# Fused local attention, gated mixing and a channel block on one core: spatial weights turned by VectorE, gate and projection later, the last v products first

## The reference

```
a = softmax(scale * q k^T + bias, masked to 8 global keys and a window of 96)   per head
x = a v                                      (B, S, 512), heads side by side

h = relu(x @ w_in)                           (B, S, 1024)
u, v = h[..., :512], h[..., 512:]
v_n = (v - mean(v)) / sqrt(var(v) + 1e-6)
v_s = einsum('ts,bsd->btd', w_spatial, v_n) + b_spatial      (mixes positions)
x = (u * v_s) @ w_out

h = x^T @ U @ V  (rank 32);  u = x + h^T
out = u + relu(u @ w_ch1) @ w_ch2            (hidden width 2048)
```

## Time and profile before

| | us |
|---|---|
| median of 3 runs (lowest, highest) | 562.88 (561.1, 563.14) |
| the profiled execution | 561.43 |
| its span, first to last instruction | 559.6 |
| TensorE busy | 525.5 (94%) |
| VectorE busy | 292.0 (52%) |
| ScalarE busy | 172.2 (31%) |
| GpSimd busy | 112.1 (20%) |

### The profile page before, as it was taken

The page is one execution under the profiler, slowest core; times in us unless marked ns, Lnnn a source line. Parts: engine busy times, 40 slices in busy tenths (PEclk is TensorE's granted clock), DMA queues, the critical chain, the costliest instruction groups (busy, mean ns, idle before and its releaser), DMA issues.

```text
span 559.6 us, 7557 instructions
## 1 busy us (share of the span) xinstructions
PE 525.5 (94%) x2676; PEld 409.6 (73%) x2676; DVE 292.0 (52%) x848; ACT 172.2 (31%) x426; POOL 112.1 (20%) x134
## 2 busy tenths in 40 slices
PE   1778999989999999999989999999999999999996
PEld 0455666567777788878768888888888888888885
DVE  4778888867775535689822265523146524011112
ACT  2665665555555533232311101021110102111010
POOL 3886000000000001499389500000000000000000
PEclk9999999999999999999989999999999999999999
DMA  8996453555514100055223100002000002000002
GB/s 176 220 222 131 101 103 90 119 113 131 127 48 123 29 29 1 1 170 166 79 75 114 37 1 0 1 0 76 0 1 1 1 0 77 0 1 0 1 0 81
DMA packets 43979, 37.04 MB, mean 66 GB/s; under 512 B 25600, under 2 KB 37888, under 8 KB 43936
## 3 DMA queue, kind: packets, MB, share of 16 engines
q1 hardware_dynamic: 37920, 20.13, 16.8%
q0 software_dynamic: 3216, 11.63, 6.8%
q10 hardware_dynamic: 2800, 4.72, 2.9%
HBM read 33.33 MB, written 3.15 MB: 65 GB/s over the span
## 4 chain that ended last, share of the span: by engine, by line
PE 80%; DVE 9%; DMA 3%; POOL 3%; issue 3%; ACT 1%; SPq 0%; DVEq 0%; POOLq 0%; ACTq 0%
PE ps L1185 66%; PE ps L1177 5%; PE ps L1225 4%; PE ps L1200 4%; DMA w_raw<-in_moe_w_in 3%; DVE uT_first L1003 2%; POOL win_lo L433 2%; PE ps L1316 1%; DMA qk_even<-in_q 1%; POOL win_hi L431 1%; DVE pr L875 1%; DVE uT_lo L1010 1%; DVE wspT_lo L962 1%; DVE gv_lo L943 1%; DVE sc L859 1%
## 5 line engine op out<-in xcount | busy, mean ns | idle before, releaser
L1123 DVE SCALAR_TENSOR_TENSOR hT_lo<-ps,hT_hi 128x512 fp32r<-128x512 f32 x48 | 33.2, 692 | 171.4 <-ACT hT_hi L731 171.4
L731 ACT ACTIVATE hT_hi<-ps 128x512 fp32r<-128x512 f32 x48 | 28.7, 598 | 228.3 <-PE ps L1185 228.3
L557 ACT ACTIVATE pr<-sc,small 128x256 f32<-128x256 f32 (+1 forms) x96 | 46.2, 483 | 52.5 <-DVE small L859 52.0
L1200 PE MATMUL ps<-k_turned,q_turned 64*128 64x256 f32 (+1 forms) x192 | 35.4, 448 | 16.5 <-DVE k_turned L811 10.0
L859 DVE CUSTOM_DVE_ANT_0 sc<-ps,bias 128x256 f32<-128x256 f32 (+1 forms) x96 | 34.9, 399 | 19.7 <-PE ps L1200 16.3
L1185 PE MATMUL ps<-win_hi,xT_hi 128*128 128x512 f32 x96 | 39.9, 416 | 0.0
L1003 DVE STREAM_TRANSPOSE ys<-tokens 32x128 f32<-32x128 f32 x128 | 38.7, 302 | 1.8
L1185 PE MATMUL ps<-uT_hi,w1a_hi 128*128 128x512 f32 x96 | 38.0, 396 | 1.0 <-DVE uT_lo L1010 1.0
L1185 PE MATMUL ps<-uT_hi,w1a_lo 128*128 128x512 f32 x96 | 38.1, 396 | 0.0
L1185 PE MATMUL ps<-uT_lo,w1a_hi 128*128 128x512 f32 x96 | 38.0, 396 | 0.0
L1185 PE MATMUL ps<-win_hi,xT_lo 128*128 128x512 f32 x96 | 37.7, 393 | 0.0
(11 more groups left out here) (146 smaller groups left out, 1078.0 us busy)
## 6 DMA issues: line engine op xcount, KB each, us to landing
w_raw<-in_moe_w_ch POOLq DMA_DIRECT2D x16, 512.0 KB, 4.0
wsp<-in_moe_w_spatial ACTq DMA_DIRECT2D x12, 384.0 KB, 3.5
vn<-in_v SPq DMA_DIRECT2D x12, 256.0 KB, 3.8
out<-ys SPq DMA_DIRECT2D x12, 256.0 KB, 3.3
qk_late<-in_q SPq DMA_DIRECT2D x24, 112.0 KB, 3.5
qk_late<-in_k SPq DMA_DIRECT2D x24, 112.0 KB, 3.9
vp<-in_v SPq DMA_DIRECT2D x10, 224.0 KB, 4.5
w_raw<-in_moe_w_in POOLq DMA_DIRECT2D x4, 512.0 KB, 7.1
```

What stands on the lines that cost most here:

```text
L557: act.activation(pr[:, k % 3, e, 0:w], sc[:, k % 2, e, 0:w], ACT.Exp, bias=nmax[:, k % 2, e:e + 1], scale=-1.0, accum_out=sums[:, k % 3, e ...
L731: act.activation(hT[0][:, n % 2, :], h1_ps(n), ACT.Relu).then_inc(s["hT_hi"], 1)
L1123: dve.scalar_tensor_tensor(hT[1][:, n % 2, :], h1_ps(n), 0.0, hT[0][:, n % 2, :], ALU.max, ALU.subtract).then_inc(s["hT_lo"], 1)
L1200: pe.matmul(scores_ps(e)[:, 0:w], q_turned[rows, tile % 2, p, :], keys[:, window_at(i):window_at(i) + w]).then_inc(s["scores"], 1)
```

## The change

- w_spatial is loaded in another layout: four transfers a tile (load_wsp), each of 32 partitions with 24 runs of 32 numbers (128 bytes), so that 32 x 32 block turns give its transpose. VectorE turns a half tile (128 x 384) with one instruction (turn_wsp) into wsp_turned, an SBUF tile that shares the place of wspT's low half. wsp_hi and wsp_lo read it there (SBUF minus SBUF, in place). TensorE's wsp_transpose is gone, and with it the PSUM banks that it used.
- In the second batch odd tiles have a home of their own for the raw and for the turned weights (wsp_late, wspT_late, wsp_turned_late), so loads run one tile further ahead.
- Freed banks: the transposed probabilities alternate between two until unit 31 (before: 24), x between two until tile 8 (PAIRED; before: 6).
- In the window stage TensorE makes gate_transpose after the second unit of a tile, and the projection after the third. VectorE's gT_lo stands behind its third unit, x2_lo behind its first, the turns of the next tile's weights on both sides of its second; ScalarE's lists follow.
- The v products of tiles 4 and 5 of batch 1 come first, then their u products (u_v_late).
- Tokens 0 and 1 are turned among the layer norms of batch 1 (eight turn_tokens calls), tokens 2 and 3 in products(1), two calls a tile instead of four; uT_hi and uT_lo come one tile earlier. In products(1) VectorE turns and splits the weights of tile t+1 ahead of gate t.
- finish(): hidden(0) goes ahead of the low rank product of tile 4.

```diff
-        wsp = sb("wsp", [P, S])
+        wsp = sb("wsp", [P, TURNS, NT, TURN])
...
-            return ps[:, 4 + (k % 2 if k < NT * NP else 0), :].rearrange("p (e c) -> p e c", e=2)
+            return ps[:, 4 + (k % 2 if k < ALONE else 0), :].rearrange("p (e c) -> p e c", e=2)
...
-            return ps[:, 6 + (tile % 2 if tile < NT else 0), :]
+            return ps[:, 6 + (tile % 2 if tile < PAIRED else 0), :]
...
+        def wsp_second(b, t):
+
+            return b == B - 1 and t % 2 == 1
...
-        wsp_d = w_sp.rearrange("(i p) s -> i p s", p=P)
+        wsp_d = w_sp.rearrange("(i r a) (k y c) -> i y r (a k) c", a=TURNS, r=TURN, y=TURNS, c=TURN)
...
-            def load_wsp(t):
-                act.dma_start(wsp[:, :], wsp_d[t, :, :]).then_inc(s["wsp_loaded"], 16)
+            def load_wsp(b, t):
+                for y in range(TURNS):
+                    act.dma_start(wsp_in(b, t)[y * TURN:(y + 1) * TURN, :, :, :].rearrange("p a k c -> p (a k) c"),
+                                  wsp_d[t, y, :, :, :]).then_inc(s[f"wsp_loaded{int(wsp_second(b, t))}"], 16)
...
+            def wsp_hi(b, t, h):
+                act.wait_ge(s["wsp_turned"], b * (2 * NT) + 2 * t + h + 1)
+                half = slice(h * HALF, (h + 1) * HALF)
+                act.activation(wspT_of(b, t)[0][:, half, :], wsp_turned_of(b, t)[:, half, :], ACT.Copy).then_inc(s["wspT_hi"], 1)
...
                 for t in range(NT):
                     a, after = ALONE + 3 * t, (t + 1) // NT
+                    exps(a + 2)
                     if t:
                         x2_hi(0, t - 1, False)
-                    exps(a + 2)
                     probs_out(a)
-                    gT_hi(0, t)
+                    if a + 2 > LAST:
+                        gT_hi(0, t)
                     exps(a + 3)
+                    wsp_hi(after, (t + 1) % NT, 0)
                     probs_out(a + 1)
-                    wsp_hi(after, (t + 1) % NT, 0, False)
+                    if a + 2 <= LAST:
+                        gT_hi(0, t)
                     exps(a + 4)
-                    wsp_hi(after, (t + 1) % NT, 1, False)
-                    load_wsp((t + 2) % NT)
+                    wsp_hi(after, (t + 1) % NT, 1)
+                    if t + 2 <= NT:
+                        load_wsp((t + 2) // NT, (t + 2) % NT)
...
+            def turn_wsp(b, t, h):
+                m = b * NT + t
+                half = slice(h * HALF, (h + 1) * HALF)
+                if h == 0:
+                    loads = sum(wsp_second(n // NT, n % NT) == wsp_second(b, t) for n in range(m + 1))
+                    dve.wait_ge(s[f"wsp_loaded{int(wsp_second(b, t))}"], 16 * TURNS * loads)
+                    dve.wait_ge(s["mixed"], m - 1 if b and t else m)
+                dve.transpose(wsp_turned_of(b, t)[:, half, :].rearrange("p k (r a) -> p a k r", a=TURNS),
+                              wsp_in(b, t)[:, :, half, :]).then_inc(s["wsp_turned"], 1)
...
+                dve.tensor_tensor(wspT_of(b, t)[1][:, half, :], wsp_turned_of(b, t)[:, half, :], wspT_of(b, t)[0][:, half, :],
+                                  ALU.subtract).then_inc(s["wspT_lo"], 1)
...
-                    gate(b, t, True)
-                    for h in range(2):
-                        if t + 1 < NT:
-                            wsp_lo(b, t + 1, h, True)
-                    for x in range(2):
-                        if b and t < TB:
-                            turn_tokens(t, x)
+                    if b == 0:
+                        gate(b, t, True)
+                    if t + 1 < NT:
+                        for h in range(2):
+                            turn_wsp(b, t + 1, h)
+                        for h in range(2):
+                            wsp_lo(b, t + 1, h)
+                    if b:
+                        gate(b, t, True)
+                        if t < TB:
+                            for g in (8 + 2 * t, 9 + 2 * t):
+                                turn_tokens(g // TURNS, g % TURNS)
                     if t:
                         x2_lo(b, t - 1, True)
                     gT_lo(b, t)
-                    for x in range(2, TURNS):
-                        if b and t < TB:
-                            turn_tokens(t, x)
-                    if b and t >= 2:
-                        uT_lo(0, t - 2)
+                    if b and 0 < t <= TB:
+                        uT_lo(0, t - 1)
...
+                    if k in (22, 24):
+                        turn_wsp(0, 0, (k - 22) // 2)
...
                 for t in range(NT):
                     a, after = ALONE + 3 * t, (t + 1) // NT
+                    unit(a, True)
                     if t:
                         x2_lo(0, t - 1, False)
-                    unit(a, True)
                     turn_next(a)
                     gate(0, t, False)
+                    turn_wsp(after, (t + 1) % NT, 0)
                     unit(a + 1, True)
-                    gT_lo(0, t)
+                    turn_wsp(after, (t + 1) % NT, 1)
                     turn_next(a + 1)
-                    wsp_lo(after, (t + 1) % NT, 0, False)
+                    if a + 2 > LAST:
+                        gT_lo(0, t)
+                    wsp_lo(after, (t + 1) % NT, 0)
                     if a + 2 <= LAST:
                         unit(a + 2, True)
+                        gT_lo(0, t)
                         turn_next(a + 2)
-                    wsp_lo(after, (t + 1) % NT, 1, False)
+                    wsp_lo(after, (t + 1) % NT, 1)
...
                     layer_norm(1, t)
+                    if t <= TB:
+                        for g in (2 * t - 2, 2 * t - 1):
+                            turn_tokens(g // TURNS, g % TURNS)
...
+            def u_v_late(b, t, wide):
+                for q in (0, 1):
+                    u_v_piece(b, t, q, wide)
+                for q in (2, 3):
+                    if t == NT - 1:
+                        u_v_piece(b, t - 1, q, wide)
+                for q in (2, 3):
+                    if t != NT - 2:
+                        u_v_piece(b, t, q, wide)
...
                 for t in range(NT):
-                    a, after = ALONE + 3 * t, (t + 1) // NT
+                    a = ALONE + 3 * t
                     mix_tokens(0, t, False)
                     unit(a)
-                    gate_transpose(0, t)
+                    if a + 2 > LAST:
+                        gate_transpose(0, t)
                     unit(a + 1)
+                    if a + 2 <= LAST:
+                        gate_transpose(0, t)
+                    if t == 1:
+                        wait(pe, "xT_lo", PAIRED)
                     if t:
                         low_rank(0, t - 1, False)
-                    wsp_transpose(after, (t + 1) % NT, 0, False)
-                    project(0, t, False)
-                    wsp_transpose(after, (t + 1) % NT, 1, False)
                     if a + 2 <= LAST:
                         unit(a + 2)
+                    project(0, t, False)
...
                 products(1)
-                wait(pe, "wspT_lo", 2 * B * NT)
+                hidden(0)
                 low_rank(1, NT - 2, True)
-                hidden(0)
                 project(1, NT - 1, True)
```

More of the change, by code:

```diff
@@ L63 @@
 CREDIT = dict(qk_turned=1, bias_ready=1, scores=1, biased=1, exps=4, normal=1, probsT=3,
-              pT_ready=2, av=1, xT_hi=1, xT_lo=2, d_xT_lo=3, v_relu=2, u_relu=2, wsp_transposed=1, wspT_lo=2, gate=2,
+              pT_ready=2, av=1, xT_hi=1, xT_lo=2, d_xT_lo=3, v_relu=2, u_relu=2, gate=2,
               gT_lo=1, x2_split=2, low_rank=2, mix_split=1, h_ps=1, u_ready=2, h1_ps=1,
@@ L175, in program @@
         wspT = hi_lo("wspT", [P, NT, P])
+        wspT_end = place[0]
+        place[0] = wspT_at + NT * P * 4
+        wsp_turned = sb("wsp_turned", [P, NT, P])
+        assert place[0] == wspT_end
         vf_at = place[0]
@@ L298, in program @@
             xT_hi xT_lo uv v_done u_relu v_relu stats_ready meanvar_ready var_ready rstd_ready normed
-            gv_hi gv_split wsp_transposed wspT_hi wspT_lo mixed gate gate_transposed gT_hi gT_lo
+            gv_hi gv_split wsp_turned wspT_hi wspT_lo mixed gate gate_transposed gT_hi gT_lo
             x2_sum x2_hi x2_split low_rank mix_hi mix_split h_ps u_ready
@@ L754, in _ @@
         def _(dve):
-            give(dve, "qk_turned", "bias_ready", "biased", "normal", "xT_lo", "d_xT_lo", "wspT_lo", "gate", "gT_lo",
+            give(dve, "qk_turned", "bias_ready", "biased", "normal", "xT_lo", "d_xT_lo", "gate", "gT_lo",
                  "x2_split", "mix_split", "u_ready", "hT_lo", "y_ready")
@@ L1051, in every @@
                     for h in range(2):
-                        wsp_lo(b, 0, h, True)
+                        turn_wsp(b, 0, h)
+                    for h in range(2):
+                        wsp_lo(b, 0, h)
                     for t in range(NT):
                         layer_norm(b, t)
+                        if b and 0 < t <= TB:
+                            for g in (2 * t - 2, 2 * t - 1):
```

(35 more changed lines are left out.)

73 lines of the change are left out of this document (44 added, 29 removed).

## The result

The changed kernel takes **570.9 us** (570.3 to 572.0, four runs) beside 562.7 us of the kernel before: ratio 1.0153, 95% interval 1.0128 to 1.0178. It is slower by 1.5%. The profiled execution took 570.92 us, span 569.1.

What follows compares the result with a forecast made beforehand. From 118.5 us on the kernel was taken as a chain of TensorE instructions, where only TensorE time and pauses count. The terms, -1.5 + 7.1 + 0 + 0.9 = +6.5 us, gave 568.5 us, range 560 to 576.

Steps and rivals of the forecast that it cites:

- term 2: Before the first mix at 118.5: xT_lo wait and transposes go, VectorE gets two turns; -1.5 us (-2.7 to 0).
- term 5: Second batch's products: 6.9 us of transposes and waits removed, 7.8 us added; +0.9 us (-6.9 to +7).
- term 3: First batch's products: waits for VectorE and a late load add 10.75 us, transposes remove 3.6; +7.1 us (0 to +16).
- Term 1: TensorE's weight transposes removed: 0.6 us a tile, 3.6 us in the first batch's products, 2.4 us in the second's.
- Term 4: Second batch's u and v products: VectorE gets 10 us of token turns and is full; TensorE's time changes by 0.
- (a): Second batch's products: last gv_lo late by VectorE's full queue in the u and v stage, 1.5 us (0 to 3.5).
- (b): Second batch's products: gate 0 stands behind two turns and two wspT_lo of tile 1; TensorE waits 2.7 us.
- (c): Second batch's products: wspT_lo, both operands in SBUF, blocked by GpSimd's splits, 1.3 us a tile; gated waits of 3.6 us.
- Clock: Second batch's products: half clock behind the x_lo and uT_lo waits moves behind two new waits, 0 (-1.5 to +2).
- (A): Second batch freed, not slower, if VectorE's list stays under TensorE's 8.0 us a tile: -2.8 us, 559.3; chance 0.2.
- (B): Loads of short runs late in every tile, not tile 0 alone: 7 us more, 576 us; chance 0.13.
- (C): Nearly cancels: turns take 0.55 us, little blocking; first batch's products +4, second's -1.5, in all +1: 563.5 us; chance 0.12.

Runs made afterwards that it cites:

- e1: Changed kernel with the first batch's gate transposed after a tile's first unit and projected before its third, gT_lo ahead of the second turn: 562.8 us, ratio 1.0013.
- e4: Changed kernel with each tile's raw weights loaded as before, one transfer of 3 KB rows (output not the reference's): 570.3 us, ratio 1.0153.
- e7: Changed kernel with the first batch's gate transposed and gT_lo taken early, but the projection still behind the third unit: 569.8 us, ratio 1.0141.
- e6: As e5, with two of the eight token turns moved from the second batch's layer norms into its products: 556.4 us, ratio 0.9895.
- e3: Changed kernel with the turned weights of the second batch's tiles 1 to 5 in PSUM instead of SBUF: 565.7 us, ratio 1.0063.
- e5: Changed kernel with the edits of e1 and e3 together: 558.3 us, ratio 0.9913.
- e8: Kernel before with only the second batch's last two v products put ahead of their u products: 560.0 us, ratio 0.9957.
- e10: Kernel before with only the first batch changed, in the order of e1: 557.8 us, ratio 0.9926.

## Why the prediction was right, step by step

The forecast was 568.5 us and slower; 570.9 is 2.4 above it and inside the range. The mechanism held in both places; several sizes were off. By the traces the change adds 9.5 us where my terms summed to 6.5 (8.2 by the medians): term 2 came out 0.5 too hopeful and term 5 3.0 too low, term 3 was 0.7 too high, and inside the terms too much and too little partly cancelled, which is luck.

**Term 1, the transposes' price, 0.6 us a tile: too low.** Tile 2 of e1, without a wait in either kernel, takes 13.28 us where it took 14.00 (e1's mixes start at 145.64 and 158.92): 0.72. In the second batch, the stage's 67.0 us are the 63.1 of before, less 4.4 us of waits that it had, plus 10.6 of new ones and 1.6 of half clock, which leaves 3.9 for the transposes where I had 2.4. That is a remainder, but five tiles at 0.72 make 3.6. Together they were worth about 2 us more than my 6.0.

**Term 2, -1.5 us: -1.0 in the table, sign and mechanism held.** From TensorE's pause at 91 us, which both traces have, to the first mix it is 27.5 us before and 26.15 in the changed kernel (118.52 - 91.04 and 117.51 - 91.36), -1.3. The wait of 2.0 us for xT_lo is gone, as forecast. A wait of 0.5 us for the scores, right ahead of the mix, is new and took back part of the relief; that VectorE's two turns cause it is not shown, they stand at 91.6 and 98.4.
The four rows, before and then changed:
```profile
91.04 0.63 PE L1177 MATMUL ps<-ident,pr 128*128 128x128 f32 x4 [0.48 <-issue]
...
118.52 0.50 PE L1185 MATMUL ps<-gv_hi,wspT_hi 128*128 128x512 f32 x1
```
```profile
91.36 0.63 PE L1247 MATMUL ps<-ident,pr 128*128 128x128 f32 x4 [0.48 <-issue]
...
117.51 0.50 PE L1255 MATMUL ps<-gv_hi,wspT_hi 128*128 128x512 f32 x1
```

**Term 3, +7.1 us: +6.4 measured, and tile by tile.** Beside the kernel before the tiles took +5.1, +0.1, +0.1, +0.2, +1.6 and -0.8 us; the forecast was +4.7 (3.2 + 0.9 + 1.2 - 0.6), +0.35 twice, +0.65, +1.7 and -0.6. The projection of tile 1 was put at M + 7.25 and came at M + 7.19. Tile 4 is right to 0.1. Tile 0's size is right in good part by luck. The wait for the scores was 0.85 smaller than forecast, and 1.6 us of half clock behind the waits of 2.35 and 0.73 were not in the sum. The raw weights, to which I gave 1.2 us, were not late at all: VectorE's turn follows gated at once, and each of the four transfers landed a median 3.5 us after its issue, where I had 6.7 for the tile. The new load does cost tile 0 1.2 us, as e4 shows, but through ScalarE's queue, whose issuing I had put at 0. And e7 shows that I named the lesser of two causes: I worked out when gT_lo comes, but not that the projection, moved behind the third unit, no longer covers that unit's operands.

**Term 4, 0: held.** The stage took 34.6 us in both. VectorE's time went from 17.9 to 23.3 us there.

**Term 5, +0.9 us: +3.9 measured.** This is where the forecast fell short.
(a) The last gv_lo was to cost 1.5 us (0 to 3.5). It cost 1.26 + 3.46 = 4.7, outside my bounds. From VectorE's first addition to its last gv_lo it is now 31.2 us where it was 27.3. VectorE is busy for 26.7 of them, close to the 27.1 that I had summed; the other 4.5 us are the short waits of each layer norm, which I named and did not put into the size. Both last steps of the chain are slow, vnf 1.24 us (0.55 in the other tiles) and gv_lo 2.05 (0.68), beside GpSimd's first splits. But they were as slow in the kernel before, 1.24 and 2.09, so they are no part of the difference. e6 took half of this wait away by moving two token turns, which shows the queue's part. The stretch in the changed kernel and its vnf, then the vnf of the kernel before:
```profile
217.03:248.23 31.20, 26.54 (x116) 21.32 (x114) 26.71 (x65) 7.98 (x14) 8.28 (x8) 0.96 0.00 1
...
244.25 1.24 DVE L993 TENSOR_SCALAR vnf<-vf,small 128x512 f32<-128x512 f32 x1 [0.44 <-POOL small L485]
```
```profile
234.84 1.24 DVE L950 TENSOR_SCALAR vnf<-vf,small 128x512 f32<-128x512 f32 x1 [0.44 <-POOL small L455]
```
(b) Gate 0: 2.7 us forecast, 3.6 measured. The turns cost what I said (1.5), the two wspT_lo 3.2 instead of 1.0, as my own part (c) should have told me.
(c) The block by GpSimd: 1.3 us a tile forecast, 9.3 us in five tiles measured, 1.9 each. The mechanism is the one I named, and e3 shows it by moving one operand. Four tiles are blocked, by 1.9 to 3.0 us, and the fifth hardly, and the mean of wspT_late_lo is 1216 ns, well over 0.55, as was said to show it. The waits for gated of tiles 1 to 3 came to 2.3 us and not 3.6: I had put TensorE's list at 8.0 us, and half clock made it longer, 3.2 us of extra time in this stage, which may be the reason; no run tells. The block is the rule of the Trainium skill, page SBUF — State Buffer, section Who interferes with whom, which the forecast cited: the traces agree, with 3.17 us for a pair beside a split and 1.02 for the same pair with an operand in PSUM. The forecast's way without that rule would have missed by 3.6 us more.
Clock: I had taken the loss as moved, 0 (-1.5 to +2). Fourteen products and the first transposes of gated ran at half clock, 3.2 us, against some nine products, 1.6 us, before: +1.6.
So the sum of term 5 was short by 2.8 us of waits and 1.6 of clock, and the transposes gave back 1.5 more than it had: 0.9 + 2.8 + 1.6 - 1.5 = 3.8.

**The rivals.** (A), the second batch freed, needed less than 0.5 us blocked a tile; it was 1.9. With that block gone and the first batch in e1's order the changed kernel is faster than the one before: e5 by 4.9 us, e6 by 6.8. (B), loads of short runs, is refuted by e4: 0.6 us in all, within the noise. The page DMA: Bandwidth & Descriptors of the Trainium skill, Specifications, stood on its side; the packets do cost the DMA engines twice the time, but the queues had room. (C) had the sign of the sum and no more: a turn takes 0.75 us and not 0.55, and its term 5 was to be -1.5.

**What was said to show it.** Mixes every 14.12 and 14.14 us in tiles 1 and 2 (14.2 forecast), with 0.65 us for gT_lo (0.95); in tile 3, which I had put beside them, 14.55. Scores in tile 0: 2.35 (3). No wait of VectorE for raw weights, against one in tile 0: wrong. gv_lo and gated head the waits of the second batch; the first hidden product waits for nothing: both right.

## What to carry to other kernels

When work moves from the bound engine to one with room, ask what now stands between each pair of its results and their use: here, with the same turns, the first batch's products took 6.4 us more than before or 1.3 less, by whether gT_lo and the 2.85 us projection stood ahead of the third unit's work or behind it. Look at the destination engine stage by stage and not as a mean: the turns paid in the first batch (1.1 to 1.3 us won, with the projection in place) and lost in the second, where 44 of 53 us were taken and a third engine shared the operands' memory. And where VectorE must work beside GpSimd's splits, keep one operand in PSUM: 1.02 us a pair here instead of 2.9 to 4.0.

## What the runs showed of the hardware that I had not expected

- VectorE turns 128x384 faster into PSUM than within SBUF: 562 ns against 874 ns a piece, in one kernel (e3). I had looked for the effect of the operand, not of the output.
```profile
L1011 DVE STREAM_TRANSPOSE wsp_turned<-wsp 128x384 f32<-128x384 f32 x14 | 12.1, 874 | 0.0
...
L1011 DVE STREAM_TRANSPOSE ps<-wsp_late 128x384 f32<-128x384 f32 x6 | 3.1, 562 | 0.0
```
- The half clock (1.2 instead of 2.4 GHz) behind a wait is not certain. After the same wait for xT_lo (1.95 and 1.96 us), the kernel before ran on at full clock and took 4.4 us to the first mix; e8, with the same instructions there, took 6.0 with the clock at 0.72. The same holds for the waits for x_lo and uT_lo: half clock in the kernel before, full clock in e8 and e10. What decides is open; one profiled execution can hold 1.6 us of it or not. First the kernel before, then e8:
```profile
114.00:118.60 4.60, 4.50 (x35) 2.98 (x35) 3.12 (x13) 2.75 (x8) 0.55 (x1) 1.00 1.03 218
```
```profile
114.00:120.20 6.20, 6.01 (x35) 4.08 (x35) 3.22 (x15) 3.01 (x8) 0.55 (x1) 0.72 0.82 182
```
- ScalarE's queue took 2.76 us to issue four of the new transfers in a row in the changed kernel, where I had charged nothing for issuing. The copy behind them was due: that of the first v of the second batch starts 5.7 us into its stage, 3.1 in e4, but VectorE had room for it, and the stage takes 34.6 us in both.
```profile
208.01 2.76 ACTq L573 DMA_DIRECT2D wsp<-in_moe_w_spatial  x4
210.82 0.60 ACT L633 ACTIVATE vf<-ps 128x512 f32<-128x512 f32 x1 [4.04 <-issue]
```
In tile 0 of the first batch it was not free. The mix starts at 117.5 us in the changed kernel and in e4, but the four transfers hold gv_hi back by 1.8 us; VectorE's gv_lo and all behind it come later, and the mix waits 0.4 us for gv_lo. The changed kernel, then e4:
```profile
117.54 2.09 ACTq L573 DMA_DIRECT2D wsp<-in_moe_w_spatial  x3
...
120.18 0.62 ACT L641 ACTIVATE gv_hi<-vnf 128x512 fp32r<-128x512 f32 x1
```
```profile
118.35 0.62 ACT L640 ACTIVATE gv_hi<-vnf 128x512 fp32r<-128x512 f32 x1
```
